# Two blocks instead of six in the loop body of the expert stage of a Hyena and MLP kernel

## The chip, the cores and the metric

The kernel runs on one core of a Trainium2 chip. A core has TensorE (PE: matmuls and transposes, its weight loads are shown as PEld), VectorE (DVE), ScalarE (ACT), GpSimd (POOL) and SyncE (SP), which issues the DMAs. Each engine runs its own program from first to last instruction and waits for the others by semaphores. The metric is device microseconds of one execution.

## The reference, cut to what matters

```python
def _attn_ref(x, v, pos_emb, w1, w2):            # x, v: (2, 12480, 128)
    h_filt = (np.maximum(pos_emb @ w1, 0.0) @ w2) * window
    u = x * v
    y = irfft(rfft(u, 2 * S) * rfft(h_filt, 2 * S))[:, :S]   # long convolution over the sequence
    return x * y

def _moe_ref(x, w_in, w_out, a, b):              # 24960 tokens, 128 -> 2048 -> 128
    h = x @ w_in
    P = a[0] + a[1] * h + a[2] * h**2 + a[3] * h**3
    Q = 1.0 + np.abs(b[0]) * np.abs(h) + np.abs(b[1]) * h**2
    return (P / (Q + 1e-06)) @ w_out
```

## The kernel before

There are three stages, each a `Block` in which every engine has a program of its own. The fold stage (to about 240 us) multiplies x by v, computes the filter and does the first half of a two-step Fourier transform. The inverse stage (to about 600 us) multiplies in the frequency domain and transforms back. The last stage, the expert stage, finishes the inverse transform, multiplies by x and runs the MLP with the rational function. Only this one is changed. The first two have loops as well: five passes of six blocks, and twelve passes of eight steps.

The expert stage works through 30 blocks (`J_BLOCKS`) of 4 x 104 = 416 tokens for each of the two batch entries. The hidden layer has 16 tiles of 128; two of them make a pair, so a block has 2 x 8 = 16 pairs (`BLOCK_PAIRS`), and the stage has 480. For one pair the engines do this:

- TensorE: `hidden` (six float32r matmuls of split operands into `h_p`, for the pair six ahead, `LEAD_H`), and `project` (two float32 matmuls of `g_s` into `acc_p`).
- ScalarE: `logarithm` and `reciprocal` (1/Q as exp(-ln Q)), then `magnitude` (half of |h|) and `squared`, both for the pair four ahead (`LEAD_E`).
- VectorE: `magnitude` (the other half), `activation` (writes `g_s`), `numerator`; once for each batch entry `sums` copies `acc_p` to `oT`, which TensorE awaits before it starts to fill `acc_p` again.
- GpSimd: `slopes` (`slope` from `mag`) and `dens` (`den` from `slope` and `mag`).

Between the pairs, at fixed places m of a block (`UNFOLD`, `TIMES_X`, `TURN_IN`, `SPLIT_HI`, `SPLIT_LO`, `SUMS`, `TURN_OUT`, `LEAVE`), stands the work that prepares the next block and stores the last one. The order is written out by hand; nothing reorders it. Each engine runs `step(i, q, ...)` for q from 0 to `PER` - 1 in three copies: iteration 0 in straight code, iterations 1 to `ITERS` - 2 in a `Fori` loop (a branch back at its end, on each engine for itself and with no barrier), and the last iteration in straight code again. `PER` is 96 pairs (`BLOCKS` = 6) and `ITERS` 5, so the loop body runs three times and branches back twice. The branches are at L643 (GpSimd), L727 (ScalarE), L837 (VectorE) and L936 (TensorE).

Of the kernel before, what the change touches and what calls it, by code (L numbers as in the profile page):

```python
# [26 lines left out]
BATCH, SEQ, D = 2, 12480, 128  # L27
# [12 lines left out]
J_BLOCKS = J // JB  # L40
# [33 lines left out]
def hyena_mlp(nc, x, v, pos_emb, w1, w2, w_in, w_out, a, b, tab, out):  # L74
# [30 lines left out]
    with ExitStack() as whole:  # L105
# [431 lines left out]
        with ExitStack() as ctx:  # L537
# [4 lines left out]
                return ctx.enter_context(nc.psum_tensor(name, shape, F32))  # L542

            BLOCK_PAIRS = BATCH * PAIRS
            BLOCKS = 6
            PER = BLOCKS * BLOCK_PAIRS
            ITERS = J_BLOCKS // BLOCKS
            LEAD_H, LEAD_E, DEEP, NUMS, SQUARES = 6, 4, 4, 8, 2
            HALF = JB // 2
            vin_s = sb("vin_s", [K1, SLOTS, JB, 2, BD])  # L550
# [42 lines left out]
            @block.sync  # L593
            def _(sp):
                def load(blk, s):
                    if positive(blk - 1):
                        sp.wait_ge(rows_done, (blk - 1) * 2)
                    sp.dma_start(vin_s[:, s].rearrange("p j c f -> p j (c f)"),
                                 back[bass.ds(blk * JB, JB)].rearrange("j k f -> k j f")).then_inc(vin_in[s], 16)
                    if positive(blk - 1):  # L600
                        sp.wait_ge(xy_done, (blk - 1) * 2)
                    sp.dma_start(x_s[:, s], x_r[:, :, bass.ds(blk * JB, JB), :]).then_inc(x_in[s], 16)

                def store(blk, b_):
                    sp.wait_ge(o_done, blk * BATCH + b_ + 1)
                    sp.dma_start(out_r[b_, :, bass.ds(blk * JB, JB), :], o_s[:, b_]).then_inc(stored[b_], 16)

                load(0, 0)
                load(1, 1)
                with sp.Fori(0, J_BLOCKS // SLOTS - 1) as i:  # L610
                    for s in range(SLOTS):
                        load((i + 1) * SLOTS + s, s)
                        for b_ in range(BATCH):
                            store(i * SLOTS + s, b_)
                for s in range(SLOTS):
                    for b_ in range(BATCH):
                        store(J_BLOCKS - SLOTS + s, b_)
                for b_ in range(BATCH):
                    sp.wait_ge(stored[b_], 16 * J_BLOCKS)
# [33 lines left out]
            def _(act):  # L653
# [47 lines left out]

                def step(i, q, more, ahead):

                    blk, m = i * BLOCKS + q // BLOCK_PAIRS, q % BLOCK_PAIRS
                    if ahead or q + 1 < PER:
                        logarithm(i + (q + 1) // PER, (q + 1) % PER)
                    reciprocal(i, q)
                    if m in LEAVE:
                        c = blk * BATCH + LEAVE.index(m) - 1
                        s = (LEAVE.index(m) + 1) % BATCH  # L710
                        if positive(c + 1):
                            act.wait_ge(turned_o, c + 1)

                            before = blk if s == 0 else blk - 1
                            if positive(before):
                                act.wait_ge(stored[s], before * 16)
                            nc.scalar.activation(o_s[:, s], m_p[0:ROWS].rearrange("p (j d) -> p j d", j=JB),
                                                 ACT.Copy).then_inc(o_done, 1)
                    if ahead:
                        from_h(i + (q + LEAD_E) // PER, (q + LEAD_E) % PER)  # L720
                    if more and m in SPLIT_HI:
                        half = SPLIT_HI.index(m)
                        split_hi((blk + 1) * 2 + half, (q // BLOCK_PAIRS + 1) % SLOTS, half)
# [4 lines left out]
                    for q in range(PER):  # L728
                        step(i, q, True, True)
                for q in range(PER):  # L730
                    step(ITERS - 1, q, q < PER - BLOCK_PAIRS, q + LEAD_E < PER)
                c = J_BLOCKS * BATCH - 1
                act.wait_ge(turned_o, c + 1)
                act.wait_ge(stored[1], (J_BLOCKS - 1) * 16)
# [3 lines left out]
            def _(dve):  # L738
# [77 lines left out]
                    numerator(0, q)  # L816

                def step(i, q, more, ahead):
                    blk, m = i * BLOCKS + q // BLOCK_PAIRS, q % BLOCK_PAIRS
                    nxt, s = (blk + 1) * 2, (q // BLOCK_PAIRS + 1) % SLOTS  # L820
                    if ahead:
                        magnitude(i + (q + LEAD_E) // PER, (q + LEAD_E) % PER)
                    activation(i, q)
                    if m in SUMS:
                        c = blk * BATCH + SUMS.index(m) - 1
                        if positive(c + 1):
                            sums(c)
                    if more and m in TIMES_X:
                        times_x(nxt + TIMES_X.index(m), i * (BLOCKS // SLOTS) + (q // BLOCK_PAIRS + 1) // SLOTS, s, TIMES_X.index(m))
                    if ahead:  # L830
                        numerator(i + (q + LEAD_E) // PER, (q + LEAD_E) % PER)
                    if more and m in SPLIT_LO:
                        split_lo(nxt + SPLIT_LO.index(m), s, SPLIT_LO.index(m))
# [4 lines left out]
                    for q in range(PER):  # L838
                        step(i, q, True, True)
                for q in range(PER):  # L840
                    step(ITERS - 1, q, q < PER - BLOCK_PAIRS, q + LEAD_E < PER)
                sums(J_BLOCKS * BATCH - 1)

            @block.tensor
            def _(pe):
# [18 lines left out]
                def hidden(i, q):  # L864
                    G = i * PER + q
                    if q % BLOCK_PAIRS == 0:
                        pe.wait_ge(lo_done, (i * BLOCKS + q // BLOCK_PAIRS + 1) * 2)
                    if positive(G - 1):
                        pe.wait_ge(num_done, G - 1)
                    s, b_ = q // BLOCK_PAIRS % SLOTS, q // PAIRS % BATCH  # L870
                    for t in range(2):
                        at = ((q % PAIRS) * 2 + t) * 128
                        for n, (w, f) in enumerate(((w_lo, xy_hi), (w_hi, xy_hi), (w_hi, xy_lo))):
                            mm = nc.tensor.matmul(h_p[:, q % 2, t, 0:TOK], w[:, at:at + 128], f[:, s, b_, :],  # L874
                                                  start=(n == 0), stop=(n == 2))
                    mm.then_inc(h_done, 1)

                def project(i, q):
                    G = i * PER + q
                    pe.wait_ge(act_done, G + 1)  # L880
                    if q % PAIRS == 0 and positive(G):
                        pe.wait_ge(oT_done, i * BLOCKS * BATCH + q // PAIRS)
                    for t in range(2):
                        ft = (q % PAIRS) * 2 + t
                        mm = nc.tensor.matmul(acc_p[:, 0:TOK], w_out_k[:, ft], g_s[:, q % DEEP, t], start=(ft == 0),  # L885
                                              stop=(ft == FT - 1))
                    mm.then_inc(used[q % DEEP], 1)
# [6 lines left out]
                    mm.then_inc(turned_o, 1)  # L894

                def step(i, q, more, ahead):
                    blk, m = i * BLOCKS + q // BLOCK_PAIRS, q % BLOCK_PAIRS
                    project(i, q)
                    nxt, s = (blk + 1) * 2, (q // BLOCK_PAIRS + 1) % SLOTS
                    if more and m in TURN_IN:  # L900
                        turn_in(nxt + TURN_IN.index(m))
                    if ahead:
                        hidden(i + (q + LEAD_H) // PER, (q + LEAD_H) % PER)
                    if more and m in UNFOLD:
                        half = UNFOLD.index(m)

                        def freed():
                            if half:
                                pe.wait_ge(lo_done, nxt + 1)
                            elif positive(blk * BATCH):  # L910
                                pe.wait_ge(o_done, blk * BATCH)

                        rows(nxt + half, i * (BLOCKS // SLOTS) + (q // BLOCK_PAIRS + 1) // SLOTS, s, half, freed)
                    if m in TURN_OUT:
                        c = blk * BATCH + TURN_OUT.index(m) - 1
                        if positive(c + 1):

                            def freed():
                                if TURN_OUT.index(m) and more:
                                    pe.wait_ge(lo_done, nxt + 2)  # L920
                                elif positive(c):
                                    pe.wait_ge(o_done, c)

                            turn_out(c, freed)
# [12 lines left out]
                    for q in range(PER):  # L937
                        step(i, q, True, True)
                for q in range(PER):
                    step(ITERS - 1, q, q < PER - BLOCK_PAIRS, q + LEAD_H < PER)  # L940
                turn_out(J_BLOCKS * BATCH - 1, lambda: pe.wait_ge(o_done, J_BLOCKS * BATCH - 1))

# [19 lines left out]
```

## Time and profile before

| | |
|---|---|
| median of 3 runs | 2110.04 us (2109.18 to 2115.88) |
| the profiled execution | 2115.88 us, its span 2114.1 us |
| mean granted TensorE clock | 0.983 |
| busy | PE 94%, PEld 69%, DVE 86%, ACT 86%, POOL 89% |
| expert stage | from about 610 us to the end, 480 pairs |
| instructions | 33,039 |

The profile lists for each engine how long its instructions ran, in order of time or grouped by line, and for idle time before one the instruction of another engine that ended last among those it depends on.
### The profile page before, as it was taken

To read this page: it belongs to the slowest core of one execution; us is meant where nothing else is said; L and a number is where in the kernel's file an instruction comes from. 1 tells how busy PE (TensorE), PEld (TensorE's weight loads), DVE (VectorE), ACT (ScalarE), POOL (GpSimd) and SP (SyncE) were. 2 spreads that over 40 slices of the span, in tenths; PEclk is the share of its full clock that TensorE was granted. 3 is DMA by queue.
4 is the path that set the end of the run, shared out by engine and by line. 5 is a ranking of instruction groups with operands and counts; after the bars stand their busy time and mean duration, and the time that the engine had idled before them with its cause. 6 is when DMAs were issued, how large, how long until landed. Compare 5 with 4: busy or idle time off the path is not lost. (4 is left out here: it accounts for less than half of the span.)

```text
span 2114.1 us, 33039 instructions
## 1 busy us (share of the span) xinstructions
PE 1985.2 (94%) x8964; PEld 1467.0 (69%) x8964; DVE 1827.0 (86%) x2511; ACT 1826.1 (86%) x2671; POOL 1872.4 (89%) x1218
## 2 busy tenths in 40 slices
PE   6999499999969999999999999999999999999998
PEld 4767399999956666666666666666666666666664
DVE  4888488888848999999999989999899999999997
ACT  4888466666638999999999999999999999999998
POOL 3777388888829999999999989999999999999997
PEclk9999799999979999999999999999999999999999
DMA  6999856776650111111111111111111111111100
GB/s 172 299 303 313 229 141 171 182 176 171 165 124 2 36 32 32 41 48 34 32 32 32 32 33 32 32 36 32 33 32 47 44 32 32 32 32 32 32 13 13
DMA packets 65843, 176.34 MB, mean 83 GB/s; under 512 B 5046, under 2 KB 8414, under 8 KB 62686
## 3 DMA queue, kind: packets, MB, share of 16 engines
q1 hardware_dynamic: 65694, 174.67, 30.6%
q8 instruction: 55, 0.90, 0.2%
q14 instruction: 94, 0.77, 0.1%
HBM read 102.89 MB, written 71.76 MB: 83 GB/s over the span
## 5 line engine op out<-in xcount | busy, mean ns | idle before, releaser
L636 POOL TENSOR_TENSOR den<-slope,mag 128x832 f32<-128x832 f32 x480 | 947.9, 1975 | 0.0
L885 PE MATMUL acc_p<-g_s,w_out_k 128*128 128x416 f32 x1920 | 769.5, 523 | 49.6 <-DVE oT L807 24.5
L766 DVE SCALAR_TENSOR_TENSOR num<-square,level,h_p 128x832 f32<-128x832 f32 x480 | 518.1, 1079 | 83.0 <-ACT square L674 43.6
L628 POOL TENSOR_SCALAR slope<-mag,den_c 128x832 f32<-128x832 f32 x480 | 499.8, 1041 | 80.6 <-DVE mag L761 51.1
L885 PEld LDWEIGHTS acc_p<-g_s,w_out_k 128*128 128x128 f32 x1920 | 341.5, 189 | 296.2 <-issue 183.5
L799 DVE SCALAR_TENSOR_TENSOR g_s<-num,ratio,r_p 128x832 f32<-128x832 f32 x480 | 518.1, 1079 | 20.3 <-ACT r_p L690 5.8
L674 ACT ACTIVATE square<-h_p,centre 128x832 f32<-128x832 f32 x480 | 470.5, 980 | 41.8 <-issue 21.0
L874 PE MATMUL h_p<-xy_hi,w_lo 128*128 128x416 f32 x960 | 460.8, 480 | 7.1 <-DVE num L766 4.5
L683 ACT ACTIVATE den<-den 128x832 f32<-128x832 f32 x480 | 442.9, 923 | 6.9 <-POOL den L636 6.8
L690 ACT ACTIVATE r_p<-den 128x832 f32<-128x832 f32 x480 | 428.6, 893 | 0.9 <-DVE g_s L799 0.7
L874 PE MATMUL h_p<-xy_lo,w_hi 128*128 128x416 f32 x960 | 338.6, 353 | 0.0
L874 PE MATMUL h_p<-xy_hi,w_hi 128*128 128x416 f32 x960 | 338.0, 352 | 0.0
L761 DVE TENSOR_SCALAR mag<-h_p 128x416 int32<-128x416 int32 x480 | 280.4, 584 | 9.8 <-PE h_p L874 9.5
L666 ACT ACTIVATE mag<-h_p 128x416 f32<-128x416 f32 x480 | 260.1, 542 | 4.4 <-PE h_p L874 4.4
L874 PEld LDWEIGHTS h_p<-xy_hi,w_lo 128*128 128x128 f32 x960 | 182.2, 190 | 107.7 <-DVE num L766 80.3
L421 POOL TENSOR_TENSOR bin_lo<-bin_s,bin_hi 120x768 fp32r<-120x768 f32 x96 | 178.3, 1857 | 67.5 <-ACT bin_hi L440 67.5
L213 POOL TENSOR_TENSOR uh_lo<-uh,uh_hi 104x768 fp32r<-104x768 f32 x60 | 151.6, 2546 | 77.6 <-ACT uh_hi L244 77.5
L874 PEld LDWEIGHTS h_p<-xy_hi,w_hi 128*128 128x128 f32 x960 | 183.3, 191 | 49.9 <-issue 38.8
L874 PEld LDWEIGHTS h_p<-xy_lo,w_hi 128*128 128x128 f32 x960 | 181.9, 190 | 1.3
L510 PE MATMUL x_p<-bin_hi,spread_lo 120*120 120x384 f32 x384 | 130.1, 339 | 27.9 <-POOL bin_lo L421 27.9
L253 ACT ACTIVATE part_s<-g_p,turn_k 96x768 f32<-96x768 f32 x120 | 107.7, 898 | 41.0 <-PE g_p L345 35.2
L853 PE MATMUL m_p<-vin_s,unfold 96*104 96x512 f32 x240 | 116.6, 609 | 15.5 <-DMA vin_s<-back 14.3
(79 smaller groups left out, 2806.3 us busy)
## 6 DMA issues: line engine op xcount, KB each, us to landing
bent<-bent_s SPq DMA_DIRECT2D x60, 576.0 KB, 6.9
bin_s<-bent SPq DMA_DIRECT2D x24, 1440.0 KB, 9.8
x_s<-in_x SPq DMA_DIRECT2D x60, 416.0 KB
back<-back_s SPq DMA_DIRECT2D x24, 960.0 KB, 7.8
vin_s<-back SPq DMA_DIRECT2D x30, 768.0 KB, 6.2
v_s<-in_v SPq DMA_DIRECT2D x30, 416.0 KB
out<-o_s SPq DMA_DIRECT2D x60, 208.0 KB
pos_s<-in_pos_emb SPq DMA_DIRECT2D x30, 88.0 KB
```

Source lines behind the costliest of these rows:

```text
L421: nc.gpsimd.tensor_tensor(bin_lo[:, q % BINS], bin_s[:, s, m], bin_hi[:, q % BINS].bitcast(F32), ALU.subtract).then_inc(bin_lo_done, 1)
L628: nc.gpsimd.tensor_scalar(slope[:, q % DEEP], mag[:, q % DEEP], den_c[:, 1:2], den_c[:, 0:1], ALU.mult, ALU.add).then_inc(slope_done, 1)
L636: nc.gpsimd.tensor_tensor(den[:, q % DEEP], slope[:, q % DEEP], mag[:, q % DEEP], ALU.mult).then_inc(den_done, 1)
L666: nc.scalar.activation(mag[:, q % DEEP, 0], h_p[:, q % 2, 0, 0:TOK], ACT.Abs).then_inc(mag_act, 1)
L674: nc.scalar.activation(square[:, q % SQUARES], h_p[:, q % 2, :, 0:TOK], ACT.Square, bias=centre[:]).then_inc(square_done, 1)
L683: nc.scalar.activation(den[:, q % DEEP], den[:, q % DEEP], ACT.Ln, bias=1.0 + EPS).then_inc(log_done, 1)
L690: nc.scalar.activation(r_p[:, :, 0:TOK], den[:, q % DEEP], ACT.Exp, scale=-1.0).then_inc(r_done, 1)
L761: nc.vector.tensor_scalar(mag[:, q % DEEP, 1].bitcast(I32), h_p[:, q % 2, 1, 0:TOK].bitcast(I32), NO_SIGN, None, ALU.bitwise_and).then_inc ...
L766: nc.vector.scalar_tensor_tensor(out=num[:, q % NUMS], in0=square[:, q % SQUARES], scalar=level[:], in1=h_p[:, q % 2, :, 0:TOK], op0=ALU.a ...
L799: nc.vector.scalar_tensor_tensor(out=g_s[:, q % DEEP], in0=num[:, q % NUMS], scalar=ratio[:, 0:1], in1=r_p[:, :, 0:TOK], op0=ALU.add, op1= ...
L874: mm = nc.tensor.matmul(h_p[:, q % 2, t, 0:TOK], w[:, at:at + 128], f[:, s, b_, :], start=(n == 0), stop=(n == 2))
L885: mm = nc.tensor.matmul(acc_p[:, 0:TOK], w_out_k[:, ft], g_s[:, q % DEEP, t], start=(ft == 0), stop=(ft == FT - 1))
```

## The change

The expert stage's loop body holds `SLOTS` = 2 blocks instead of `BLOCKS` = 6. `PER` goes from 96 to 32 pairs and `ITERS` from 5 to 15. The rest rewrites indices to the same values: the block number is `i * SLOTS + q // BLOCK_PAIRS`, and the last iteration prepares a next block only during its first block. Every engine executes the same arithmetic on the same tiles in the same order; what differs is how much of it stands in straight code, and how often a branch is taken.

```diff
             BLOCK_PAIRS = BATCH * PAIRS
-            BLOCKS = 6
-            PER = BLOCKS * BLOCK_PAIRS
-            ITERS = J_BLOCKS // BLOCKS
+            PER = SLOTS * BLOCK_PAIRS
+            ITERS = J_BLOCKS // SLOTS
...
-                with sp.Fori(0, J_BLOCKS // SLOTS - 1) as i:
+                with sp.Fori(0, ITERS - 1) as i:
...
-                    blk, m = i * BLOCKS + q // BLOCK_PAIRS, q % BLOCK_PAIRS
+                    blk, m = i * SLOTS + q // BLOCK_PAIRS, q % BLOCK_PAIRS
...
-                    step(ITERS - 1, q, q < PER - BLOCK_PAIRS, q + LEAD_E < PER)
+                    step(ITERS - 1, q, q < BLOCK_PAIRS, q + LEAD_E < PER)
...
-                        times_x(nxt + TIMES_X.index(m), i * (BLOCKS // SLOTS) + (q // BLOCK_PAIRS + 1) // SLOTS, s, TIMES_X.index(m))
+                        times_x(nxt + TIMES_X.index(m), i + (q // BLOCK_PAIRS + 1) // SLOTS, s, TIMES_X.index(m))
...
-                        pe.wait_ge(lo_done, (i * BLOCKS + q // BLOCK_PAIRS + 1) * 2)
+                        pe.wait_ge(lo_done, (i * SLOTS + q // BLOCK_PAIRS + 1) * 2)
```

Where the branches stand, on ScalarE. The end of the loop body before, with the first rows of the peeled last iteration behind it:

```order
L683 ACTIVATE den<-den 128x832
L690 ACTIVATE r_p<-den 128x2x416
L663 REGISTER_ALU
L666 ACTIVATE mag<-h_p 128x416
L674 ACTIVATE square<-h_p,centre 128x832
L727 REGISTER_ALU
L727 COMPARE_AND_BRANCH
```

The same place in the changed kernel, whose lines are one less:

```order
L682 ACTIVATE den<-den 128x832
L689 ACTIVATE r_p<-den 128x2x416
L662 REGISTER_ALU
L665 ACTIVATE mag<-h_p 128x416
L673 ACTIVATE square<-h_p,centre 128x832
L726 REGISTER_ALU
L726 COMPARE_AND_BRANCH
```

The instructions around the branch are the same. Before, 534 listed instructions of ScalarE lie from the loop's first to this branch, now 186 (waits that are instructions of their own are not listed). The start of the loop body before, with the end of the peeled first iteration ahead of it:

```order
L666 ACTIVATE mag<-h_p 128x416
L674 ACTIVATE square<-h_p,centre 128x832
L727 UNCONDITIONAL_BRANCH
L727 ISA
L683 ACTIVATE den<-den 128x832
L687 REGISTER_ALU
```

And now:

```order
L665 ACTIVATE mag<-h_p 128x416
L673 ACTIVATE square<-h_p,centre 128x832
L726 UNCONDITIONAL_BRANCH
L726 ISA
L682 ACTIVATE den<-den 128x832
L686 REGISTER_ALU
```

The loop starts after the same work, four listed instructions of a pair; ahead of it lie 32 pairs now, not 96. TensorE's branch before stands between `h_p` of the pair six ahead and the `acc_p` of the new iteration's first pair:

```order
L874 MATMUL h_p<-xy_hi,w_lo 128x416
L874 MATMUL h_p<-xy_hi,w_hi 128x416
L874 MATMUL h_p<-xy_lo,w_hi 128x416
L936 REGISTER_ALU
L936 COMPARE_AND_BRANCH
L885 MATMUL acc_p<-g_s,w_out_k 128x416 x2
```

And now:

```order
L873 MATMUL h_p<-xy_hi,w_lo 128x416
L873 MATMUL h_p<-xy_hi,w_hi 128x416
L873 MATMUL h_p<-xy_lo,w_hi 128x416
L935 REGISTER_ALU
L935 COMPARE_AND_BRANCH
L884 MATMUL acc_p<-g_s,w_out_k 128x416 x2
```

Here too nothing but the distance back to the loop's first instruction has changed.

## Rows read from the trace of the kernel before

**Rows 1.** The page, part 1: busy time, share of the span, instructions by engine.

```profile
PE 1985.2 (94%) x8964; PEld 1467.0 (69%) x8964; DVE 1827.0 (86%) x2511; ACT 1826.1 (86%) x2671; POOL 1872.4 (89%) x1218
```

**Rows 2.** The page, part 5: busy, mean ns of one, idle before, releaser; GpSimd.

```profile
L636 POOL TENSOR_TENSOR den<-slope,mag 128x832 f32<-128x832 f32 x480 | 947.9, 1975 | 0.0
...
L628 POOL TENSOR_SCALAR slope<-mag,den_c 128x832 f32<-128x832 f32 x480 | 499.8, 1041 | 80.6 <-DVE mag L761 51.1
```

**Rows 3.** GpSimd on `slope`, `den`, by 16 pairs: us, busy, clock, DMA share, GB/s.

```profile
1172.70:1221.30 48.60, 47.38 (x33) 1.00 0.14 35
1221.30:1274.20 52.90, 47.32 (x33) 0.97 0.13 33
1274.20:1322.90 48.70, 47.45 (x33) 1.00 0.14 35
1517.30:1570.30 53.00, 47.45 (x33) 0.97 0.13 33
1813.40:1861.90 48.50, 47.30 (x33) 1.00 0.14 34
1861.90:1910.40 48.50, 47.34 (x33) 1.00 0.13 35
```

**Rows 4.** ScalarE in order of time, first jump: start, us, instruction [idle before].

```profile
1223.88 1.00 ACT L674 ACTIVATE square<-h_p,centre 128x832 f32<-128x832 f32 x1
...
1226.69 1.02 ACT L674 ACTIVATE square<-h_p,centre 128x832 f32<-128x832 f32 x1
1230.33 0.90 ACT L683 ACTIVATE den<-den 128x832 f32<-128x832 f32 x1 [2.62 <-POOL den L636]
1231.13 0.85 ACT L690 ACTIVATE r_p<-den 128x832 f32<-128x832 f32 x1
1231.92 0.50 ACT L666 ACTIVATE mag<-h_p 128x416 f32<-128x416 f32 x1
```

**Rows 5.** The same view where the loop is left.

```profile
1818.77 1.01 ACT L674 ACTIVATE square<-h_p,centre 128x832 f32<-128x832 f32 x1
1819.61 0.95 ACT L683 ACTIVATE den<-den 128x832 f32<-128x832 f32 x1
```

**Rows 6.** All engines in order of time, first jump.

```profile
1225.32 1.99 POOL L636 TENSOR_TENSOR den<-slope,mag 128x832 f32<-128x832 f32 x1
...
1228.28 1.98 POOL L636 TENSOR_TENSOR den<-slope,mag 128x832 f32<-128x832 f32 x1
...
1232.19 1.08 DVE L799 SCALAR_TENSOR_TENSOR g_s<-num,ratio,r_p 128x832 f32<-128x832 f32 x1 [0.74 <-ACT r_p L690]
...
1232.65 1.03 POOL L628 TENSOR_SCALAR slope<-mag,den_c 128x832 f32<-128x832 f32 x1 [2.40 <-ACT mag L666]
...
1233.18 0.59 DVE L807 COPY oT<-acc_p 128x416 f32<-128x416 f32 x1
...
1233.83 2.78 PE L885 MATMUL acc_p<-g_s,w_out_k 128*128 128x416 f32 x4 [3.38 <-DVE oT L807]
...
1238.39 0.59 DVE L761 TENSOR_SCALAR mag<-h_p 128x416 int32<-128x416 int32 x1 [0.90 <-PE h_p L874]
```

**Rows 7.** Stretches: PE, PEld, DVE, ACT, POOL busy (x), granted clock, DMA share, GB/s.

```profile
1234.20:1237.60 3.40, 3.40 (x8) 2.17 (x7) 3.13 (x4) 3.21 (x5) 3.40 (x3) 0.50 0.00 0
```

**Rows 8.** The page, part 3: instruction packets, MB, share of 16 engines.

```profile
q8 instruction: 55, 0.90, 0.2%
q14 instruction: 94, 0.77, 0.1%
```

**Rows 9.** DMA queues from 1226 to 1234 us.

```profile
q14 instruction: 5, 0.04, 1.8%
q8 instruction: 2, 0.03, 1.6%
```

**Rows 10.** DMA queues from 1227 to 1229.5 us.

```profile
q14 instruction: 3, 0.02, 3.9%
```

**Rows 11.** DMA queues from 700 to 1210 us.

```profile
q8 instruction: 16, 0.26, 0.2%
q14 instruction: 25, 0.20, 0.1%
```

**Rows 12.** DMA queues from 320 to 580 us: this row is the only one.

```profile
q1 hardware_dynamic: 11462, 45.09, 67.5%
```

**Rows 13.** GpSimd in order of time at a jump of the inverse stage.

```profile
323.15 1.85 POOL L421 TENSOR_TENSOR bin_lo<-bin_s,bin_hi 120x768 fp32r<-120x768 f32 x1 [0.40 <-ACT bin_hi L440]
...
326.67 1.85 POOL L421 TENSOR_TENSOR bin_lo<-bin_s,bin_hi 120x768 fp32r<-120x768 f32 x1 [0.41 <-ACT bin_hi L440]
...
330.18 1.86 POOL L421 TENSOR_TENSOR bin_lo<-bin_s,bin_hi 120x768 fp32r<-120x768 f32 x1 [0.41 <-ACT bin_hi L440]
```

**Rows 14.** DMA queues from 1819 to 1821 us, where the loop is left.

```profile
q14 instruction: 1, 0.01, 1.0%
```

**Rows 15.** DMA queues from 1218 to 1226 us.

```profile
q14 instruction: 2, 0.02, 0.7%
```

More of the change, by code:

```diff
@@ L818, in step @@
                 def step(i, q, more, ahead):
-                    blk, m = i * BLOCKS + q // BLOCK_PAIRS, q % BLOCK_PAIRS
+                    blk, m = i * SLOTS + q // BLOCK_PAIRS, q % BLOCK_PAIRS
                     nxt, s = (blk + 1) * 2, (q // BLOCK_PAIRS + 1) % SLOTS
@@ L840, in _ @@
                 for q in range(PER):
-                    step(ITERS - 1, q, q < PER - BLOCK_PAIRS, q + LEAD_E < PER)
+                    step(ITERS - 1, q, q < BLOCK_PAIRS, q + LEAD_E < PER)
                 sums(J_BLOCKS * BATCH - 1)
@@ L866, in hidden @@
                     if q % BLOCK_PAIRS == 0:
-                        pe.wait_ge(lo_done, (i * BLOCKS + q // BLOCK_PAIRS + 1) * 2)
+                        pe.wait_ge(lo_done, (i * SLOTS + q // BLOCK_PAIRS + 1) * 2)
                     if positive(G - 1):
                         pe.wait_ge(num_done, G - 1)
-                    s, b_ = q // BLOCK_PAIRS % SLOTS, q // PAIRS % BATCH
+                    s, b_ = q // BLOCK_PAIRS, q // PAIRS % BATCH
                     for t in range(2):
@@ L881, in project @@
                     if q % PAIRS == 0 and positive(G):
-                        pe.wait_ge(oT_done, i * BLOCKS * BATCH + q // PAIRS)
+                        pe.wait_ge(oT_done, i * SLOTS * BATCH + q // PAIRS)
                     for t in range(2):
@@ L896, in step @@
                 def step(i, q, more, ahead):
-                    blk, m = i * BLOCKS + q // BLOCK_PAIRS, q % BLOCK_PAIRS
+                    blk, m = i * SLOTS + q // BLOCK_PAIRS, q % BLOCK_PAIRS
                     project(i, q)
@@ L911, in freed @@
                                 pe.wait_ge(o_done, blk * BATCH)
-                        rows(nxt + half, i * (BLOCKS // SLOTS) + (q // BLOCK_PAIRS + 1) // SLOTS, s, half, freed)
+                        rows(nxt + half, i + (q // BLOCK_PAIRS + 1) // SLOTS, s, half, freed)
                     if m in TURN_OUT:
@@ L939, in _ @@
                 for q in range(PER):
-                    step(ITERS - 1, q, q < PER - BLOCK_PAIRS, q + LEAD_H < PER)
+                    step(ITERS - 1, q, q < BLOCK_PAIRS, q + LEAD_H < PER)
                 turn_out(J_BLOCKS * BATCH - 1, lambda: pe.wait_ge(o_done, J_BLOCKS * BATCH - 1))
```

## The prediction

> **What bounds the kernel now.** The change touches only the last stage, so I first looked for the engine that sets its pace. Over the whole span four engines are 86 to 94% busy [rows 1], which decides nothing. The groups of instructions do: a pair of f tiles costs GpSimd 1,041 + 1,975 = 3,016 ns [rows 2]. One pair passes every 3.04 us (48.6 us for the 16 pairs of one block, below), so GpSimd is the bound, with the waits for `mag` as its only idle time. ScalarE is close behind: from its square at 1223.88 to its next at 1226.69 are 2.81 us [rows 4], and twice in 16 pairs it has an output copy or a split on top.
>
> Next I cut the stage into stretches of 16 pairs [rows 3]. They take 48.5 to 48.7 us, except two: 52.9 us from 1221.3 and 53.0 us from 1517.3. GpSimd's busy time in them is the same 47.3 to 47.5 us. These are the two places where the `Fori` loops of this stage jump back: 5 times 96 pairs are one peeled copy, three passes of a loop (two jumps back) and a peeled tail. At 1813.4 the loop is left without a jump, and that stretch has 48.5 us. So a jump back costs 52.9 - 48.6 = 4.3 and 53.0 - 48.6 = 4.4 us, 4.35 on average, and leaving or entering a loop costs nothing.
>
> Then the instructions at the first jump. ScalarE ends its square at 1227.71 and starts the next logarithm, whose input GpSimd had finished before, at 1230.33, 2.62 us idle [rows 4]. The view blames GpSimd's `den`, but the one in question was written from 1225.32 to 1227.31; the one that ended at 1230.26 is the next [rows 6]. At the exit the same square and logarithm follow each other without a gap (1818.77, 1819.61) [rows 5]. The rest follows from ScalarE: its late `mag` leaves GpSimd idle for 2.40 us; its late `r_p` makes `g_s` start at 1232.19, so `oT` at 1233.18, and TensorE, which waits for that to reuse `acc_p`, stands 3.38 us [rows 6]. TensorE's granted clock then falls to 0.50 from 1234.2 to 1237.6 [rows 7], the 1.2 GHz level, its `h_p` comes late, and VectorE's next mag waits 0.90 us for it [rows 6]. That is how 2.4 becomes 4.35.
>
> What ScalarE waits for is code. The trace has a kind of DMA packet named instruction: 55 packets for 0.90 MB on q8, 16 KB each, and 94 for 0.77 MB on q14, 8 KB each [rows 8]. Between 1226 and 1234 there are two and five of them [rows 9]; of the five, three fall between 1227 and 1229.5 [rows 10]. In straight code from 700 to 1210 us there are 16 and 25 in 510 us [rows 11]. TensorE's 16 KB come once in 32 us, in which it goes through some 255 of the 2,363 instructions of a pass of 296 us (counts of the built program, below), so I read 16 KB as 256 instructions and 8 KB as 128: the three other engines' 1,998 instructions of one pass (below) need 15.6 such packets in 296 us, and 25 in 510 us are 14.5, near enough. The stall is a fetch of the loop's head, which is no longer on the engine.
>
> **When is the head still there?** The inverse-transform stage answers part of it. Its TensorE loop has 192 matmuls and as many weight loads, 384 instructions and 27 others, so it lies in at least two 16 KB packets. From 320 to 580 us, nine passes of eight steps of 3.51 us, no instruction packet at all is moved [rows 12]. And GpSimd's step over the jump at 327.7 is 3.51 us, as its neighbour: 326.67, 330.18 from 323.15 and 326.67 [rows 13]. A jump whose target is held costs nothing there.
>
> **The change, part by part.**
> The number of iterations goes from 5 of 96 pairs to 15 of 32. The first and the last stay peeled, so the loop now runs 13 times and jumps back 12 times, against 2. No arithmetic, tile or semaphore changes, and each jump still stands at the end of a block's last pair.
> The built programs give the loop bodies, in instructions, before and after: GpSimd 483 and 163, ScalarE 825 and 281, VectorE 690 and 232, TensorE 2,363 and 793 (each matmul counted with its weight load, float32 ones twice).
> GpSimd: 163 instructions, two or three 8 KB packets. VectorE: 232, also two or three. ScalarE: 281, three or four. To tell which, I use the exit of the old loop: between 1819 and 1821 one 8 KB packet is fetched [rows 14], just when ScalarE passes its branch, so its branch (the 825th instruction) lies within a few instructions of a packet's start, and the loop's head at about instruction 72 of a packet. The new peeled copy is 723 - 251 = 472 instructions shorter, which moves the head to 72 - 472 + 512 = 112 and the branch to 112 + 280 = 392 = 3 x 128 + 8. So ScalarE's new loop touches four packets, and its branch is in the fourth. Entering the fourth also fetches the fifth ahead. The head survives only if five packets of 8 KB are held.
> No row here shows an engine on 8 KB packets that holds more than two and the one ahead; TensorE held at least that many of its own. I take ScalarE's head as lost, at each of the 12 jumps. The others' heads I take as held, but this changes little: at the old jump GpSimd, VectorE and TensorE all waited behind ScalarE [rows 6].
>
> Price of a jump: at most what it costs now, 4.35 us. At least the 2.40 us that GpSimd stood for the late `mag` [rows 6], if the second round (TensorE's pause and clock) goes. I take 3.9, near the upper end, because the chain from `r_p` to `oT` to TensorE needs only ScalarE to be late; the 0.45 is off because the old fetch stood in a crowd of three packets within 2.5 us [rows 10], one of them probably ScalarE's own next page, and the new one does not.
> Sum: 12 x 3.9 = +46.8; two old jumps go, -2 x 4.35 = -8.7; eight more blocks of 16 pairs run in loop code, which is 48.6 against 48.5 us in the tail [rows 3], +0.6. Together +38.7 us. On the profiled execution, 2115.9 us (span 2114.1), that is 2154.6; on the median of 2110.0, which lies 5.8 us under it, 2148.7. I say 2149.
>
> The Trainium skill ("Runtime: NRT & Kernel Launch", Instruction fetch mechanics) says a taken branch out of the current two-page window forces a fetch before execution goes on. The trace agrees on the stall, but its TensorE loop of 411 instructions, with no packet in 260 us, shows more than one page held behind the current one or a very lucky placing. By a strict two-page window every engine would miss, and the price would be the full 4.35 us: +44.1.
>
> **The rivals.**
> *All heads held.* If ScalarE keeps five packets, all 12 jumps are as free as in the inverse stage. Then only the old price goes: -8.7 + 0.6 = -8.1 us, 2102, faster. It decides at 281 instructions against ScalarE's store. For it: the inverse and fold stages jump freely. Against it: their ScalarE loops have 62 and 128 instructions only, and GpSimd at 483 instructions already fetches at its own jump, two packets between 1218 and 1226 [rows 15]. The same section of that page gives most engines room for 512 instructions and TensorE for 2,048; read plainly, every new body fits and this rival is the page's own outcome. Chance 0.13.
> *ScalarE holds, TensorE misses.* Its 793 instructions touch four or five 16 KB packets. A fetch such as ScalarE's would cost between nothing, hidden by `h_p` being computed six pairs ahead, and 2.4 us a jump: -8.1 to +20.7, at 2102 to 2131. Chance 0.07.
> *Only the first round is paid.* With the other three on time the pipeline catches up: 12 x 2.4 - 8.7 + 0.6 = +20.7, 2131. For it: the queue ahead of GpSimd is four deep. Against it: its slack at the jump is 2.62 - 2.40 = 0.22 us. Chance 0.15.
> *Full price or more.* 12 x 4.35 - 8.1 = +44.1, 2154, and 2158 at 4.7 us a jump. Chance 0.20.
> My forecast has 0.45.
>
> **How the numbers follow.** What this kernel's measurement can tell from no change is 0.3%, 6.3 us. The three cases with a ScalarE fetch (0.80) are all slower by 20 us or more; half of the TensorE case is slower too. Faster takes 0.10 of the first rival, the rest of it and of the TensorE case are within 0.3%. So faster 0.11, same 0.06, slower 0.83. The range for 8 in 10 runs from 2122 (half way into the TensorE case) to 2158.
>
> **What would show it.** Right: stretches of 32 pairs of 97.2 + 3.9 us, 12 gaps of some 2.4 us before ScalarE's logarithm at L682, GpSimd idle behind ACT mag, 8 KB packets at each jump and half-clock dips of TensorE after it. The 16 KB packets in the loop then tell whether TensorE's head is held. Wrong: stretches of 97.2 us throughout and no instruction packets in the loop (all held), or packets but no GpSimd idle time (the fetch is hidden), which would fell the step that ScalarE is the one that costs.

## The result, and the profile after

The changed kernel took 2127.32 us (median of 6 runs, 2123.67 to 2133.15) beside 2111.72 us for the kernel before: 1.007 times as long, 95% interval 1.0057 to 1.0084. It is slower, as forecast, but by 15.6 us and not by 39. The profiled execution took 2124.51 us, its span 2122.7 us.

The page of the changed kernel, parts 1, 3 and 5:

```profile
PE 1981.8 (93%) x8964; PEld 1464.9 (69%) x8964; DVE 1825.9 (86%) x2511; ACT 1826.5 (86%) x2671; POOL 1872.6 (88%) x1218
...
q14 instruction: 83, 0.67, 0.1%
q8 instruction: 16, 0.26, 0.0%
...
L635 POOL TENSOR_TENSOR den<-slope,mag 128x832 f32<-128x832 f32 x480 | 947.9, 1975 | 0.0
...
L627 POOL TENSOR_SCALAR slope<-mag,den_c 128x832 f32<-128x832 f32 x480 | 500.1, 1042 | 91.9 <-DVE mag L760 50.0
```

GpSimd's two groups are what they were [rows 2]. The instruction packets are not: TensorE's 16 KB ones went from 55 to 16, the 8 KB ones only from 94 to 83 [rows 8]. Between 840 and 2010 us, 12 passes of the loop, there are 57 small ones and no big one (the row of the kernel's own transfers is left out):

```profile
q14 instruction: 57, 0.47, 0.1%
```

So TensorE held its loop's head, and one of the other three engines did not. 57 in 12 passes are nearly five a pass, which fits the four packets of ScalarE's body and the one ahead of them, all fetched anew in each pass. GpSimd's work on `slope` and `den` by blocks of 16 pairs (us, busy, granted clock, DMA share, GB/s), every second with a jump:

```profile
1125.50:1175.80 50.30, 47.40 (x33) 1.00 0.14 33
1175.80:1224.50 48.70, 47.46 (x33) 1.00 0.13 34
1224.50:1274.80 50.30, 47.28 (x33) 1.00 0.13 33
```

They answer to the 48.6 and 52.9 us of [rows 3]. All 12 blocks with a jump look like this, 50.3 to 50.6 us, 21.2 us above 12 times 48.6 together, so one jump costs 1.77 us. It was forecast at 3.9. One of them in order of time (start, us, instruction, idle time before):

```profile
1130.92 1.02 ACT L673 ACTIVATE square<-h_p,centre 128x832 f32<-128x832 f32 x1
...
1133.38 0.90 ACT L682 ACTIVATE den<-den 128x832 f32<-128x832 f32 x1 [1.44 <-issue]
...
1135.70 1.03 POOL L627 TENSOR_SCALAR slope<-mag,den_c 128x832 f32<-128x832 f32 x1 [1.23 <-ACT mag L665]
...
1136.22 0.58 DVE L806 COPY oT<-acc_p 128x416 f32<-128x416 f32 x1
...
1136.86 1.66 PE L884 MATMUL acc_p<-g_s,w_out_k 128*128 128x416 f32 x4 [2.19 <-DVE oT L806]
```

The chain has the links of [rows 4, 6], each shorter: ScalarE idle 1.44 us, not 2.62; GpSimd 1.23, not 2.40; TensorE 2.19, not 3.38. Over the 12 jumps ScalarE's idle time is 1.43 to 1.74 us, GpSimd's 1.21 to 1.50 (1.30 on average) and TensorE's 2.18 to 2.48. And the clock stays up where it fell before [rows 7]:

```profile
1133.00:1137.00 4.00, 1.81 (x9) 1.27 (x8) 2.33 (x5) 3.62 (x6) 2.77 (x3) 1.00 0.01 2
1137.00:1141.00 4.00, 4.00 (x18) 2.83 (x19) 3.83 (x5) 3.83 (x7) 4.00 (x3) 1.00 0.01 2
```

At a jump, from 1127 to 1140 us, four small packets move, where five small and two big did within 8 us before [rows 9]:

```profile
q14 instruction: 4, 0.03, 0.7%
```

Sum: 12 jumps +21.2, two old ones -8.7, is +12.5 us. GpSimd's stage, from the start of its first `den` to the start of its last, is 11.5 us longer (1463.0 to 1474.5). Its first block ran 1.3 us shorter, which does not look like the change's doing: that block takes 50.5 us in e1 and 49.1 in e2 and e10 below. The two profiled executions differ by 8.6 us only, because the stage also began 3.0 us earlier (634.5 and 637.4). The medians differ by 15.6; the other 3 us lie in the spread of runs.

### The profile page after: what moved, and what is told of

Read it like the earlier page. It is cut to its first block and busy times, and to the rows that moved or that the text cites. A ratio compares the mean times of both kernels' runs of the same rounds, so it can differ in the third digit from the quotient of the medians.

```text
span 2122.7 us, 33885 instructions
## 1 busy us (share of the span) xinstructions
PE 1981.8 (93%) x8964; PEld 1464.9 (69%) x8964; DVE 1825.9 (86%) x2511; ACT 1826.5 (86%) x2671; POOL 1872.6 (88%) x1218
```

## The experiments

There are two theories of when a jump costs. By the packet theory an engine keeps its loop's head if the body touches at most so many packets, hence it depends on where the body lies. By the count theory a body of more than 256 instructions loses it. The price can come from ScalarE's lateness alone, from the other engines' misses, or from TensorE's clock. (A miss is a jump whose target the engine no longer holds.) Each engine has its own loop and there is no barrier, so the number of blocks in the body can be chosen for each engine apart. Only e1 (seven runs) and e8 (four) were run more than once; the readings of the others rest on their blocks, of which those in the loop without a jump take 48.5 to 48.9 us in every kernel.

### Moving the loop by a few instructions: e1, e2, e9, e10

Four kernels are the changed kernel with n increments of an unused semaphore ahead of ScalarE's peeled first iteration, with n = 24 (e1), 8 (e2), 14 (e9), 18 (e10). They are written as the kernel before with `BLOCKS` = 2, which gives the indices the values that they have in the changed kernel, so their line numbers differ by a few. The loop is untouched, it lies n instructions later.

```diff
+                for _ in range(n):
+                    act.sem_inc(pad_act, 1)
                 for q in range(PER):
                     step(0, q, True, True)
```

e1: 

> The changed kernel with 24 semaphore increments more on ScalarE ahead of its expert-stage loop. They move the loop's head from about instruction 112 of an 8 KB instruction packet to about 8 of the next, so its 281 instructions touch three packets, not four. Packet theory (a head is held if the body touches at most three packets): no instruction packets inside the loop, every 32-pair stretch 97.2 us instead of 98.95, 12 x 1.75 = 21 us less than the changed kernel, about 2103 to 2107. Rival, count theory (a body of more than 256 instructions always loses its head, wherever it lies): unchanged, 2127, with ScalarE's gap at each of the 12 jumps.

e2: 

> The same with 8 increments instead of 24: the head goes to about instruction 120, still four packets. Packet theory: as the changed kernel, 50.3 us for each block with a jump, 2124 to 2130. A rival in which the extra instructions themselves, or any other side effect of an added row of increments, remove the stall: 48.6 us, as with 24.

e1 took 2105.74 us, 0.9967 times the kernel before (0.9955 to 0.9978), over 20 us less than the change. In its loop, 840 to 2000 us, no instruction packet moves; the one row of the queues, and two blocks, the first with a jump and the second without:

```profile
q1 hardware_dynamic: 20421, 39.15, 13.8%
```

```profile
1120.70:1169.40 48.70, 47.42 (x34) 1.00 0.14 34
1169.40:1218.00 48.60, 47.44 (x33) 1.00 0.14 34
```

From the second on, all its blocks take 48.5 to 48.7 us, and the loop's first instruction follows ScalarE's branch within 0.3 us. e2 took 2126.22 us, with 50.2 to 50.6 us at 11 of 12 jumps, as the change. The same 281 instructions cost 21 us in one place and nothing 16 instructions further on. The count theory is out.

e9: 

> As e1 with 14 increments. If ScalarE's loop head stood at instruction 112 of its packet (give or take 2, worked out before), it now stands at 126, still in the packet whose fourth successor the branch needs: 12 jumps at 1.75 us or more, about 2124 to 2130. If the head stood at 114 or later, three packets, 2105.

e10: 

> As e1 with 18 increments: the head at 130, that is instruction 2 of the next packet, the body in three packets, no fetch, about 2103 to 2108. If the head stood before 110, as the changed kernel, 2124 to 2130. Any theory in which the number of extra instructions matters other than by the packet's edge gives no such step between 14 and 18.

e10 took 2106.01 us, as e1. e9 took 2155.38 us, 25 us above the range expected and 29 above e2; the step between 14 and 18 was there, with 49 us and not 20. ScalarE at one of e9's jumps, with GpSimd and TensorE behind it:

```profile
1036.49 1.01 ACT L675 ACTIVATE square<-h_p,centre 128x832 f32<-128x832 f32 x1
...
1039.11 0.90 ACT L684 ACTIVATE den<-den 128x832 f32<-128x832 f32 x1 [1.61 <-issue]
...
1041.20 0.87 ACT L691 ACTIVATE r_p<-den 128x832 f32<-128x832 f32 x1 [1.19 <-issue]
...
1042.74 1.03 POOL L629 TENSOR_SCALAR slope<-mag,den_c 128x832 f32<-128x832 f32 x1 [2.68 <-ACT mag L667]
...
1043.90 1.61 PE L888 MATMUL acc_p<-g_s,w_out_k 128*128 128x416 f32 x2 [3.66 <-DVE oT L810]
```

ScalarE stands twice: 1.61 us before the logarithm and 1.19 us before the next instruction. With the head at instruction 126 of a packet, only two instructions come in the fetched packet. Between the stalls the trace has just these two, a register instruction of the loop and the logarithm; the third starts 1.96 us after the logarithm did. Then ScalarE needs the next packet, which comes only after the first has been entered: one 8 KB packet starts at 1037.4 us, one at 1039.6 and one at 1041.7. This places the head to the instruction: 126 - 14 = 112, as worked out from the one packet at the old loop's exit [rows 14]. GpSimd waits 2.68 us, TensorE 3.66, and the clock falls at 9 of the 12 jumps. A block with the fall, and one of the three with a jump and no fall:

```profile
1234.70:1287.90 53.20, 47.40 (x33) 0.97 0.13 31
```

```profile
1447.00:1498.70 51.70, 47.35 (x33) 1.00 0.13 32
```

Without the fall a jump costs 3.1 us, 0.5 more than GpSimd's wait of 2.6; in the change it is 0.5 more than 1.3. Seven falls last 3.4 us and their blocks take 53.1 to 53.3, two last 6.8 us and theirs take 54.1 and 54.3.

### What a jump costs, engine by engine: e3 to e7

e3 to e7 let one engine, or some, loop over six blocks and jump back twice, so that they lose their loop's head; the others loop over two. In e4 to e7 ScalarE has the increments of e1 ahead, so that in e4, e6 and e7 none of its 12 short jumps costs anything. The edit for one engine, in a kernel with `BLOCKS` = 2 (e4 has it the other way round, 2 for ScalarE alone and 6 for the rest):

```diff
             def _(act):
+                BLOCKS = 6
+                PER, ITERS = BLOCKS * BLOCK_PAIRS, J_BLOCKS // BLOCKS
```

e3, ScalarE over six: 

> ScalarE alone loops over six blocks (825 instructions, two jumps back), the other three engines over two (12 jumps each). Tells why a jump cost 4.35 us before and 1.75 in the changed kernel. If ScalarE's longer stall at the old place (head 7 packets back, its own next page fetched at the same moment) makes the price alone: 4.3 us at each of its two jumps and 48.6 elsewhere. If the price needed the misses of VectorE and TensorE: about 1.75 to 2.5 us at the two. In both cases total about 2100 to 2112.

Measured, 2112.33 us; ScalarE, GpSimd and TensorE at the first jump, then the block with it and the next:

```profile
1227.08 0.90 ACT L685 ACTIVATE den<-den 128x832 f32<-128x832 f32 x1 [2.37 <-issue]
...
1229.40 1.04 POOL L628 TENSOR_SCALAR slope<-mag,den_c 128x832 f32<-128x832 f32 x1 [2.13 <-ACT mag L668]
...
1230.56 3.14 PE L887 MATMUL acc_p<-g_s,w_out_k 128*128 128x416 f32 x4 [3.11 <-DVE oT L809]
```

```profile
1218.40:1271.00 52.60, 47.38 (x34) 0.97 0.13 32
1271.00:1319.60 48.60, 47.39 (x33) 1.00 0.14 34
```

Both jumps take 52.6 us: 4.0 us of the old 4.35 come with ScalarE's miss alone. So the low price of the change is not owed to the other engines' heads being held. What differs between e3 and the change is ScalarE's idle time, 2.37 and 1.44 us, and whether the clock falls.

e5, as e3 with 24 increments ahead: 

> ScalarE alone over six blocks, as in e3 (4.0 us a jump), with 24 increments more ahead, so that its branch stands about 24 instructions behind a packet's start, not at it. Place theory: at a packet's start the branch itself comes late and its target's fetch queues behind the next page's; away from it ScalarE's idle time before the logarithm falls from 2.37 to about 1.5 us, TensorE pauses 2.2 instead of 3.1 us, keeps its full clock, and the jump costs 1.75 us as in the changed kernel. Rival, distance theory: the head is as far back as before (7 packets), so the jump still costs 4.0 us.

Measured, 2109.53 us. The first jump and the second, then their two blocks:

```profile
1226.12 0.90 ACT L686 ACTIVATE den<-den 128x832 f32<-128x832 f32 x1 [1.48 <-issue]
...
1228.45 1.04 POOL L629 TENSOR_SCALAR slope<-mag,den_c 128x832 f32<-128x832 f32 x1 [1.24 <-ACT mag L669]
...
1229.61 1.66 PE L890 MATMUL acc_p<-g_s,w_out_k 128*128 128x416 f32 x4 [2.24 <-DVE oT L812]
```

```profile
1519.55 0.91 ACT L686 ACTIVATE den<-den 128x832 f32<-128x832 f32 x1 [1.47 <-issue]
...
1521.87 1.04 POOL L629 TENSOR_SCALAR slope<-mag,den_c 128x832 f32<-128x832 f32 x1 [1.20 <-ACT mag L669]
...
1523.04 3.14 PE L890 MATMUL acc_p<-g_s,w_out_k 128*128 128x416 f32 x4 [2.22 <-DVE oT L812]
...
1529.18 1.04 POOL L629 TENSOR_SCALAR slope<-mag,den_c 128x832 f32<-128x832 f32 x1 [1.37 <-ACT mag L669]
```

```profile
1218.30:1268.60 50.30, 47.42 (x33) 1.00 0.13 33
1511.80:1563.50 51.70, 47.46 (x33) 0.97 0.12 32
```

ScalarE's idle time fell to 1.48 and 1.47 us, so the place theory holds and the distance theory is out. In the old loop ScalarE's branch is the first instruction or so of a packet, by the count in the prediction. And the two jumps are the same to 0.05 us up to TensorE's pause of 2.24 and 2.22 us; then the clock fell to half at 1522.8 for 3.4 us at the second and stayed at the first. GpSimd waits once more, 1.37 us, and the block takes 51.7 us and not 50.3. Nothing else that the trace shows differs: the clock's fall costs 1.4 us. e2 showed it too: one of its 12 jumps, the only one with a fallen clock, took 51.67 us.

e4, the rest over six, ScalarE held: 

> The reverse: ScalarE loops over two blocks with the 24 increments (head held by the packet theory), the other three over six, with two jumps at which GpSimd, VectorE and TensorE all fetch. If ScalarE alone makes the price: 48.6 us in every block, about 2101 to 2106. If the others' misses are part of it: up to 4.35 - 1.75 = 2.6 us at each of the two places.

Measured, 2111.96 us, with VectorE, GpSimd and TensorE at the jump and its block:

```profile
1228.11 0.59 DVE L766 TENSOR_SCALAR mag<-h_p 128x416 int32<-128x416 int32 x1 [2.21 <-PE h_p L879]
...
1228.91 1.04 POOL L629 TENSOR_SCALAR slope<-mag,den_c 128x832 f32<-128x832 f32 x1 [1.54 <-DVE mag L766]
...
1230.25 3.14 PE L890 MATMUL acc_p<-g_s,w_out_k 128*128 128x416 f32 x4 [2.72 <-DVE oT L812]
```

```profile
1218.50:1270.70 52.20, 47.40 (x32) 0.97 0.13 33
```

That is 3.6 us for a jump at which ScalarE misses nothing, more than the 2.6 us allowed for. The prices do not add: ScalarE's miss alone costs 4.0 us and the others' 3.6, and all together cost 4.35, because they lie beside each other in time. e6 and e7 take the others apart.

e6, TensorE over six: 

> TensorE alone over six blocks (two fetches of its loop's head), the rest over two with ScalarE's head held. If VectorE's late mag makes the 3.6 us of e4: about 48.6 us at both places, or a few tenths more. If TensorE's branch of 3.8 us and the clock behind it make them: 2 to 3.6 us.

e7, VectorE over six: 

> VectorE alone over six blocks, the rest over two with ScalarE's head held. If VectorE's late mag makes the 3.6 us of e4: 1.5 us for GpSimd's first wait, and 3.6 in all if TensorE's clock falls behind its pause. If TensorE makes them: 48.6 us or a few tenths more.

e6 (2108.05 us), TensorE and GpSimd's later wait, and the two blocks:

```profile
1229.90 1.66 PE L890 MATMUL acc_p<-g_s,w_out_k 128*128 128x416 f32 x4 [2.55 <-issue]
...
1234.49 1.04 POOL L629 TENSOR_SCALAR slope<-mag,den_c 128x832 f32<-128x832 f32 x1 [1.43 <-ACT mag L667]
```

```profile
1218.30:1268.80 50.50, 47.36 (x33) 1.00 0.13 33
1512.00:1562.00 50.00, 47.35 (x32) 1.00 0.14 34
```

e7 (2110.17 us), the same for VectorE and GpSimd:

```profile
1226.90 0.59 DVE L766 TENSOR_SCALAR mag<-h_p 128x416 int32<-128x416 int32 x1 [2.10 <-PE h_p L879]
...
1227.69 1.04 POOL L629 TENSOR_SCALAR slope<-mag,den_c 128x832 f32<-128x832 f32 x1 [1.42 <-DVE mag L766]
...
1235.24 1.04 POOL L629 TENSOR_SCALAR slope<-mag,den_c 128x832 f32<-128x832 f32 x1 [1.45 <-ACT mag L667]
```

```profile
1217.40:1269.50 52.10, 47.37 (x32) 0.97 0.13 32
1512.70:1564.50 51.80, 47.37 (x33) 0.97 0.13 32
```

TensorE alone costs 1.9 and 1.4 us, with its clock up, which neither of e6's two expectations had. VectorE alone costs 3.5 and 3.2 us, with the clock down at both, as expected if VectorE makes the price. VectorE's miss thus explains nearly all of e4. GpSimd was not tried alone, but e4 shows its own miss apart in time. Its branch was at 1215.3 us and resumed 2.5 us later, with two 8 KB packets between 1215 and 1221, and its work went on without idle time:

```profile
1215.50 1.03 POOL L629 TENSOR_SCALAR slope<-mag,den_c 128x832 f32<-128x832 f32 x1
1216.50 1.97 POOL L637 TENSOR_TENSOR den<-slope,mag 128x832 f32<-128x832 f32 x1
1218.46 1.04 POOL L629 TENSOR_SCALAR slope<-mag,den_c 128x832 f32<-128x832 f32 x1
```

### No jump at all: e8

```diff
-            BLOCKS = 6
+            BLOCKS = 10
```

> The kernel before with ten blocks in the loop body: three iterations, one peeled at each end, so no jump back is ever taken. Every block 48.5 to 48.7 us, 8.7 us less than before, 2102 to 2107, level with e1; if code in straight line has a cost of its own (packets to fetch all the way), slower than e1.

It took 2101.38 us (2100.87 to 2101.88), 0.9955 times the kernel before (0.9938 to 0.9971), and beats both kernels.

```profile
1216.70:1265.30 48.60, 47.44 (x34) 1.00 0.14 34
```

Straight code shows no price of its own here. Its blocks take 48.5 us against 48.65 in e1's loop: 1402.2 us from the second block on against 1405.6. The likely reason is that in the loop the engines execute register instructions for their waits' values; e1's trace has one for each pair on GpSimd and more on ScalarE and VectorE, that of e8 has none. That they make the difference was not tested by itself.

## Why the prediction was right and wrong

*The mechanism* was right. The stall is a fetch of the loop's head; ScalarE's body of 281 instructions reaches some eight instructions into a fourth packet, so it alone misses (e1, e2, e9, e10). TensorE, VectorE and GpSimd held their heads, and the inverse stage was the right model for them. "All heads held" (0.13) did not come. The Trainium skill ("Runtime: NRT & Kernel Launch", Instruction fetch mechanics) gives ScalarE room for 512 instructions. The size agrees with the runs, as three packets of 128 and the one ahead are 512; but 281 were too many in this place, since whole packets are held and one of the four is the one ahead. The strict two-page window that the same section of the Trainium skill has did not come either: TensorE's 793 instructions are at least four packets of 256 by the reading made there, and none of them was fetched again. What all runs here agree with is that an engine with 8 KB packets keeps three and the one ahead.

*The step that failed* is the price of a jump, "I take 3.9": it measured 1.77. The runs show what a jump with ScalarE's miss is made of: GpSimd's wait for the late `mag`, 0.5 us more, and 1.4 us if TensorE's clock falls. The old jump was 2.40 + 0.5 + 1.4, near its 4.35; that of the change is 1.30 + 0.5, near 1.77.

Three things in the forecast were wrong. First, the 0.45 us for the old fetch's crowd was too little: away from the packet's edge ScalarE's idle time falls by 0.9 us (2.37 to 1.48, e3 to e5). Another 0.25 us went with the other engines' fetches (2.62 to 2.37, the kernel before to e3), so from the old kernel to the change it is 1.2.

Second, I wrote that "the chain from `r_p` to `oT` to TensorE needs only ScalarE to be late" and so kept the whole second round. The chain is there, but most of its price is a step that comes only with the clock: the late start alone leaves GpSimd 0.5 us more behind, and the half clock adds 1.4 us (e5, e2; 1.5 in e9). With a pause of TensorE of 3.1 us or more the clock fell at all four jumps of e3 and of the kernel before and at 9 of 12 of e9. With 2.5 to 2.7 us it fell at all four of e4 and e7, and not at the one of e6 (2.55 us). With 2.1 to 2.5 us it fell at one of 12 in e2, at one of two in e5, not at e6's other and at none of 12 in the change. [Rows 7] had shown the fall, and I did not price it apart.

Third, the lower end, 2.40 us, was taken as what GpSimd stood for the late `mag`. It was no bound, because ScalarE's stall itself could shrink; GpSimd stood 1.30 on average. The rival "only the first round is paid" (2131 us, chance 0.15) had the right shape, no second round, and came nearest; its 2.4 us a jump had the same wrong size.

*The old jumps* at 8.7 us were right. *Loop code* at +0.6 us was a little low: its own rows give 8 x 0.1 = 0.8, and e1 and e8 give 1405.6 - 1402.2 = 3.4 us for 26 blocks, 0.13 a block and 1.0 for the eight.

*"This changes little"*, said of the other engines' heads, was right for the change, since they were held, but the reason was wrong: e4 shows that they cost 3.6 us a jump when lost. In the old kernel they came late at the same time as ScalarE, and would have been late without it. The trace of the kernel before had shown it for VectorE. It stood 2.03 us before its `mag`, as it does in e7 (2.10); the view names `h_p`, but the loop's first instruction on VectorE had followed its branch only after 2.83 us, at 1230.65:

```profile
1230.85 0.59 DVE L761 TENSOR_SCALAR mag<-h_p 128x416 int32<-128x416 int32 x1 [2.03 <-PE h_p L874]
```

*The place of the head*, 112, was right to the instruction, and is the step on which the rest stood. It had little room: the prediction placed the old branch only "within a few instructions" of a packet's start, and by the same count a head nine instructions earlier would have left the body in three packets, where no jump costs anything.

## What to carry to other kernels

In these runs a branch back cost nothing where the engine still held the loop's head, and whether it does depends on where the body lies, not only on its length: count the packets that it touches, and look for packets of kind "instruction" inside the loop. A few instructions ahead of a loop can be worth 20 us, or cost 29. Where a pause may let TensorE's clock fall, price the fall by itself (here 1.4 us), and take no wait of an old stall as the least that a new one can cost.

## What the runs showed that was not expected

- A head two instructions ahead of a packet's end costs a second stall of 1.19 us, since the next packet comes only after the first is entered (e9, 2155 us against 2106 with four instructions more).
- With its branch at the start of a packet ScalarE stood 2.37 us in e3, and 24 instructions behind it 1.48 in e5. By the trace's records of branches, 0.3 of the 0.9 us is the branch itself being late (it starts 0.34 us after the instruction ahead of it, not 0.06), and 0.6 comes after it (the loop's first instruction follows it by 3.03 us, not 2.43). In the kernel before, where the other engines fetch as well, it follows by 3.28. That the fetch of the next packet, close by, makes the 0.6 us was not tested.
- The same pause of TensorE, 2.22 and 2.24 us (e5), came with half the clock for 3.4 us once and not the other time. What decides it these runs don't show.
